# Attention stage of a fused three-layer kernel: g_norm multiplied on VectorE, a second set of q/k/v buffers, weight pieces summed after a batch's additions

## What is computed

```python
kv = np.einsum('bhsd,bhse->bhde', k, v)          # per head, 64 x 64
out = np.einsum('bhsd,bhde->bhse', q, kv)
rms = np.sqrt(np.mean(out * out, axis=-1, keepdims=True) + 1e-06)
x = out / rms * g_norm                            # heads side by side: x is (8, 576, 512)
mixed = np.real(fft(fft(x, axis=1), axis=2))
u = x + mixed
# layer 1: u + relu(layernorm(u) @ w_ch1) @ w_ch2; layer 2: a mix over the sequence by U, V, then the same without the norm
```

## Time and profile before

| | |
|---|---|
| median of 3 runs | 1843.4 us (1842.77 to 1852.18) |
| profiled execution | 1847.24 us, span 1844.9 us |
| PE busy | 1744.3 us (95%), mean granted clock 0.983 |
| DVE busy | 1376.6 us (75%) |
| POOL busy | 612.4 us (33%) |
| ACT busy | 784.6 us (43%) |

### The profile page before, as it was taken

How to read it: one execution, slowest core, us unless ns; L and a number is a source line. 1 busy time by engine, 2 the same in 40 slices (tenths; PEclk the granted TensorE clock), 3 DMA queues, 4 the chain that set the end, 5 groups by cost and what they waited for, 6 DMA issues and landing times.

```text
span 1844.9 us, 25843 instructions
## 1 busy us (share of the span) xinstructions
PE 1744.3 (95%) x9908; PEld 1677.4 (91%) x9908; DVE 1376.6 (75%) x1559; ACT 784.6 (43%) x1126; POOL 612.4 (33%) x428
## 2 busy tenths in 40 slices
PE   6889879989999999999999999799999999999998
PEld 5667768979999999999999999699999999999998
DVE  4779987997777877867966868956956857758667
ACT  2333343544544544445444436334334334443442
POOL 2888973351231330330410313620400402303203
PEclk9889989999999999999999999899999999999999
DMA  7487557988787787887876779776766766767663
GB/s 254 157 277 247 203 206 272 336 326 279 261 300 270 276 290 258 293 283 254 289 250 239 259 235 344 287 262 237 242 240 232 251 227 238 249 224 247 230 244 120
DMA packets 123819, 470.04 MB, mean 255 GB/s; under 512 B 12273, under 2 KB 49649, under 8 KB 84018
## 3 DMA queue, kind: packets, MB, share of 16 engines
q1 hardware_dynamic: 122482, 467.21, 71.9%
q10 hardware_dynamic: 1216, 1.18, 0.2%
HBM read 389.70 MB, written 78.64 MB: 254 GB/s over the span
## 4 chain that ended last, share of the span: by engine, by line
PE 75%; DVE 12%; issue 4%; POOL 4%; DMA 3%; ACT 1%; SPq 1%; DVEq 0%; POOLq 0%; ACTq 0%
PE pair L841 11%; PE pair L843 11%; PE pair L842 11%; PE pair L858 11%; PE pair L860 11%; PE pair L859 11%; DVE t_raw L1370 2%; DVE t_lo L1351 2%; PE tr_ps L725 2%; PE pair L632 2%; DMA in_sb<-x_dram 1%; PE pair L653 1%; DVE w_sb L1283 1%; POOL t_raw L1576 1%; DVE eo_sb L1241 1%
## 5 line engine op out<-in xcount | busy, mean ns | idle before, releaser
L858 PE MATMUL pair<-t_hi,w_sb 128*128 128x384 f32 x1344 | 462.1, 344 | 34.2 <-DVE t_lo L1351 34.2
L841 PE MATMUL pair<-t_hi,w_sb 128*128 128x384 f32 x1344 | 460.5, 343 | 7.9 <-DVE h_sb L1388 7.1
L859 PE MATMUL pair<-t_lo,w_sb 128*128 128x384 f32 x1344 | 457.4, 340 | 0.0
L860 PE MATMUL pair<-t_hi,w_sb 128*128 128x384 f32 x1344 | 457.2, 340 | 0.0
L843 PE MATMUL pair<-t_hi,w_sb 128*128 128x384 f32 x1344 | 455.6, 339 | 0.0
L842 PE MATMUL pair<-t_lo,w_sb 128*128 128x384 f32 x1344 | 455.5, 339 | 0.0
L1351 DVE TENSOR_TENSOR t_lo<-t_raw,t_hi 128x768 fp32r<-128x768 f32 x300 | 345.4, 1158 | 13.5 <-ACT t_hi L1070 10.0
L1576 POOL TENSOR_TENSOR t_raw<-h_sb 128x768 f32<-128x768 f32 x60 | 152.0, 2534 | 575.5 <-PE pair L860 575.5
L1085 ACT ACTIVATE t_hi<-t_raw 128x768 fp32r<-128x768 f32 x240 | 202.2, 846 | 318.9 <-DVE t_raw L1370 239.4
L858 PEld LDWEIGHTS pair<-t_hi,w_sb 128*128 128x128 f32 x1344 | 254.3, 189 | 42.6 <-DVE t_lo L1351 42.3
L841 PEld LDWEIGHTS pair<-t_hi,w_sb 128*128 128x128 f32 x1344 | 252.6, 188 | 15.6 <-issue 10.2
(11 more groups left out here) (149 smaller groups left out, 2104.9 us busy)
## 6 DMA issues: line engine op xcount, KB each, us to landing
w_sb<-wc SPq DMA_DIRECT2D x260, 1024.0 KB, 4.9
wc<-w_sb SPq DMA_DIRECT2D x28, 1024.0 KB, 5.8
w_raw<-wr1a SPq DMA_DIRECT2D x24, 512.0 KB, 4.6
w_raw<-wr1b SPq DMA_DIRECT2D x24, 512.0 KB, 4.2
wc<-pb SPq DMA_DIRECT2D x16, 640.0 KB, 4.9
w_raw<-wr2a SPq DMA_DIRECT2D x10, 1024.0 KB, 7.0
wc<-pb_v SPq DMA_DIRECT2D x16, 640.0 KB, 5.2
w_raw<-wr2b SPq DMA_DIRECT2D x10, 1024.0 KB, 6.8
```

What stands on the lines that cost most here:

```text
L841: nc.tensor.matmul(ps, w_hi, hi[:, x, :], start=(fresh and x == 0), stop=False, skip_group_check=True)
L858: nc.tensor.matmul(ps, w_hi, hi[:, f, :], start=(fresh and k == 0 and f == 0), stop=False, skip_group_check=True)
L859: nc.tensor.matmul(ps, w_hi, lo[:, f, :], start=False, stop=False, skip_group_check=True)
L860: last = nc.tensor.matmul(ps, w_lo, hi[:, f, :], start=False, stop=(k == 3 and f == 1), skip_group_check=True)
```

## The change

It does three things. DVE does the multiplication by g_norm itself, directly behind each group's `normalise`, as two instructions of 96x512 in place on x_sb; POOL's `weigh` is gone. k, v and q have two sets of buffers, used by turns, and the loads wait for the last reader of two batches ago instead of the last batch; the place of the loads in SP's list changes with it: in the loop of batch b now k, v and q of b come first, then the weight pieces, then `store_u(b-2)`. Weight pieces are summed on POOL behind the batch's additions, two each for b = 1, 2, 3 and one each for b = 4, 5; ACT rounds them in the next step behind `copy_g`, DVE makes the remainder at the end of that step, and SP stores them in the loop after (`MOVED`).

```diff
+    sets = (base + 31744, base)
+    k_sb = [at(f"k_sb{r}", sets[r], [128, 5, D]) for r in range(2)]      # v_sb, q_sb alike
-        SUM_MIDDLE, SUM_END = {1: 0, 2: 2, 3: 4, 4: 5, 5: 6, 6: 7}, {1: 1, 2: 3}
-        SPLIT_EARLY, SPLIT_END = {2: 1, 3: 3}, {1: 0, 2: 2, 3: 4, 4: 5, 5: 6, 6: 7}
-        MOVED = {2: (0, 1), 3: (2, 3), 4: (4,), 5: (5,), 6: (6,), 7: (7,)}
+        SUMMED = {1: (0, 1), 2: (2, 3), 3: (4, 5), 4: (6,), 5: (7,)}
+        MOVED = {b + 2: units for b, units in SUMMED.items()}
 SP
             def load_kv(b):
+                r = b % 2
+                if b >= 2:
+                    sp.wait_ge(kv_summed, b - 1)
...
             def load_q(b):
+                if b >= 2:
+                    sp.wait_ge(att_done, 2 * NT * (b - 1))
...
-            next_kv(2)
-            load_unit(UNITS[1])
             for b in range(2, B):
-                next_q(b)
-                if b < B - 1:
-                    next_kv(b + 1)
-                for n in MOVED[b]:
+                load_kv(b)
+                load_q(b)
+                for n in MOVED.get(b, ()):
                     store_unit(UNITS[n])
                     if n + 2 < 8:
                         load_unit(UNITS[n + 2])
                 if b == 6:
-                    for q in range(NCH):
+                    for q in range(4):
                         load_in(q)
                 store_u(b - 2)
+            sp.wait_ge(att_done, 2 * NT * (B - 1))
+            for q in (4, 5):
+                load_in(q)
             store_u(B - 2)
 ACT, phase1_step(b)
-                if b in SPLIT_EARLY:
-                    split_unit_hi(UNITS[SPLIT_EARLY[b]])
                 copy_seq(b - 1, (0, 1))
                 root(b, 1)
                 copy_seq(b - 1, (2, 3))
                 copy_g(b - 1)
+                for n in SUMMED.get(b - 1, ()):
+                    split_unit_hi(UNITS[n])
                 square(b, 2, False)
...
-                if b in SPLIT_END:
-                    split_unit_hi(UNITS[SPLIT_END[b]])
 DVE, normalise(b, g)
+                for m in range(2):
+                    dve.wait_ge(scaled, 2 * (NT * b + g) + m + 1)
+                    x = x_sb[b % 3][:, 2 * g + m, :].rearrange("p (h e) -> p h e", h=H)
+                    nc.vector.tensor_tensor(x, x, gn_sb[:, :].unsqueeze(1).to_broadcast([PT, H, HD]), ALU.mult).then_inc(x_ready, 1)
 DVE, end of phase1_step(b)
-                if b in SPLIT_END:
-                    split_unit_lo(UNITS[SPLIT_END[b]])
+                for n in SUMMED.get(b - 1, ()):
+                    split_unit_lo(UNITS[n])
 POOL
-            def weigh(b, g):
...
             for b in range(1, B):
-                weigh(b, 0)
-                weigh(b, 1)
-                if b in SUM_MIDDLE:
-                    sum_unit(UNITS[SUM_MIDDLE[b]])
-                weigh(b, 2)
                 for t in range(NT):
                     add_transform(b - 1, t)
-                if b in SUM_END:
-                    sum_unit(UNITS[SUM_END[b]])
+                for n in SUMMED.get(b, ()):
+                    sum_unit(UNITS[n])
```

More of the change, by code:

```diff
@@ L183, in build_program @@
     o = base
-    k_sb = at("k_sb", o, [128, 5, D])
-    v_sb = at("v_sb", o + 10240, [128, 5, D])
-    q_sb = at("q_sb", o + 20480, [128, NP, 2 * NT * PT])
     kv_sb = at("kv_sb", o + 29696, [128, NP, 128])
[L188 to L191, removed]
+    sets = (base + 31744, base)
+    k_sb = [at(f"k_sb{r}", sets[r], [128, 5, D]) for r in range(2)]
+    v_sb = [at(f"v_sb{r}", sets[r] + 10240, [128, 5, D]) for r in range(2)]
+    q_sb = [at(f"q_sb{r}", sets[r] + 20480, [128, NP, 2 * NT * PT]) for r in range(2)]
     w_sb = [at(f"w_sb{r}", base + 8192 * r, [128, 2, 4, 2, 128], F32R) for r in range(RING)]
@@ L302, in build_program @@
         kv0_loaded, q0_loaded = [sem(f"kv0_loaded{n}") for n in range(2)], sem("q0_loaded")
-        kv_loaded, q_loaded = sem("kv_loaded"), sem("q_loaded")
+        kv_loaded, q_loaded = [[sem(f"{what}_loaded_{r}") for r in range(2)] for what in ("kv", "q")]
         kv_zeroed, warm_zeroed = sem("kv_zeroed"), sem("warm_zeroed")
@@ L404, in load_kv @@
             def load_kv(b):
[L405 to L408, removed]
+                r = b % 2
+                if b >= 2:
+                    sp.wait_ge(kv_summed, b - 1)
+                sp.dma_start(k_sb[r][:, 0:4, :], k_main[b]).then_inc(kv_loaded[r], 16)
+                sp.dma_start(k_sb[r][0:64, 4, :], k_rest[b]).then_inc(kv_loaded[r], 16)
+                sp.dma_start(v_sb[r][:, 0:4, :], v_main[b]).then_inc(kv_loaded[r], 16)
+                sp.dma_start(v_sb[r][0:64, 4, :], v_rest[b]).then_inc(kv_loaded[r], 16)
             def load_q(b):
-                sp.dma_start(q_sb[:, :, :], q_t[b]).then_inc(q_loaded, 16)
+                if b >= 2:
+                    sp.wait_ge(att_done, 2 * NT * (b - 1))
+                sp.dma_start(q_sb[b % 2][:, :, :], q_t[b]).then_inc(q_loaded[b % 2], 16)
             def load_unit(unit):
@@ L428, in _ @@
                 cols = slice(256 * n, 256 * (n + 1))
-                sp.dma_start(k0_sb[:, 0:4, cols], k_main[0][:, :, cols]).then_inc(kv0_loaded[n], 16)
-                sp.dma_start(k0_sb[0:64, 4, cols], k_rest[0][:, cols]).then_inc(kv0_loaded[n], 16)
-            sp.dma_start(q0_sb[:, :, :], q_t[0]).then_inc(q0_loaded, 16)
+                sp.dma_start(k_sb[0][:, 0:4, cols], k_main[0][:, :, cols]).then_inc(kv0_loaded[n], 16)
+                sp.dma_start(k_sb[0][0:64, 4, cols], k_rest[0][:, cols]).then_inc(kv0_loaded[n], 16)
+            sp.dma_start(q_sb[0][:, :, :], q_t[0]).then_inc(q0_loaded, 16)
             sp.dma_start(gn_sb[:, :], g_norm.partition_broadcast(PT)).then_inc(gn_loaded, 16)
@@ L440, in _ @@
             load_unit(UNITS[0])
[L442 to L448, removed]
+            load_unit(UNITS[1])
             def store_u(b):
@@ L621, in _, with kv_products @@
         def _(pe):
-            def kv_products(b, k_sb=k_sb, v_sb=v_sb, very_first=False):
-                if not very_first:
-                    pe.wait_ge(kv_loaded, 64 * b)
+            def kv_products(b):
+                r = b % 2
+                if b:
+                    pe.wait_ge(kv_loaded[r], 64 * ((b + 1) // 2))
                     pe.wait_ge(kv_copied, 2 * b)
                 for h in range(NP):
-                    if very_first and h % 2 == 0:
+                    if b == 0 and h % 2 == 0:
                         pe.wait_ge(kv0_loaded[h // 2], 64)
@@ L631, in kv_products, with attention @@
                         rows = 128 if t < 4 else 64
-                        last = nc.tensor.matmul(kv_ps[:, cols], k_sb[0:rows, t, cols], v_sb[0:rows, t, cols],
+                        last = nc.tensor.matmul(kv_ps[:, cols], k_sb[r][0:rows, t, cols], v_sb[r][0:rows, t, cols],
                                                 start=(t == 0), stop=(t == 4))
                 last.then_inc(kv_summed, 1)
-            def attention(b, groups, first, late=False, q_sb=q_sb):
+            def attention(b, groups, first, late=False):
                 if 0 in groups:
@@ L640, in attention @@
                     else:
-                        pe.wait_ge(q_loaded, 16 * b)
+                        pe.wait_ge(q_loaded[b % 2], 16 * ((b + 1) // 2))
                     pe.wait_ge(kv_copied, 2 * (b + 1))
@@ L653, in attention @@
                             last = nc.tensor.matmul(ps[0:PT, 128 * h:128 * (h + 1)],
-                                                    q_sb[:, h, PT * (2 * g + m):PT * (2 * g + m + 1)],
+                                                    q_sb[b % 2][:, h, PT * (2 * g + m):PT * (2 * g + m + 1)],
                                                     kv_sb[:, h, :], start=True, stop=True)
@@ L714, in phase1_step @@
                 feature_transform(b - 1, first)
-            kv_products(0, k0_sb, v0_sb, very_first=True)
-            attention(0, (0, 1), True, q_sb=q0_sb)
+            kv_products(0)
+            attention(0, (0, 1), True)
             kv_products(1)
-            attention(0, (2,), True, q_sb=q0_sb)
+            attention(0, (2,), True)
             for b in range(1, B):
@@ L1012, in phase1_step @@
                 copy_cos(b - 1, 2, first)
-                if b in SPLIT_END:
-                    split_unit_hi(UNITS[SPLIT_END[b]])
             for n in range(2):
                 cols = slice(256 * n, 256 * (n + 1))
-                act.dma_start(v0_sb[:, 0:4, cols], v_main[0][:, :, cols]).then_inc(kv0_loaded[n], 16)
-                act.dma_start(v0_sb[0:64, 4, cols], v_rest[0][:, cols]).then_inc(kv0_loaded[n], 16)
+                act.dma_start(v_sb[0][:, 0:4, cols], v_main[0][:, :, cols]).then_inc(kv0_loaded[n], 16)
+                act.dma_start(v_sb[0][0:64, 4, cols], v_rest[0][:, cols]).then_inc(kv0_loaded[n], 16)
             act.wait_ge(warm_zeroed, 1)
@@ L1229, in normalise @@
                         ALU.mult).then_inc(scaled, 1)
+                if b == 0 and g == 0:
+                    dve.wait_ge(gn_loaded, 16)
```

(8 more changed lines are left out.)

2 lines of the change are left out of this document (removed).

## The result

The changed kernel takes 1930.6 us (median of 4 runs, 1925.3 to 1932.0) against 1847.8 us for the kernel before (median of 4 runs): a ratio of 1.044 (95% interval 1.041 to 1.047), 83 us slower. Each kernel has one profile, so a difference of a few us between single steps rests on one execution. The direction and the mechanism were forecast; the size was not: 1900 us, range 1868 to 1925.

The account below looks back on a forecast made before the run. DVE was taken to pace the steady step. Terms of -0.7, -1.6, +11.6, +18.5, +18.5, +12.2 and -1.9 summed to +56.6 us on 1847.2, giving 1903.8, then 1900 for the median; range 1868 to 1925.

Parts of the forecast that it names:

- part 2: Place of the loads in SP's list: k and v come late, changing steps 2 to 6 by -1.6, +11.6, +18.5, +18.5, +12.2 us.
- rival B: First stage: k and v in time, ACT's wait for the weight pieces decides; 1843 us, as before; 5%.
- step 7: Stretch between marks without kv products, where only the multiplication's gain counts: -1.9 us.
- T: Time from the kv products' start to the step's mark: 15.5 us plus 2.2 for PE's slower clock, 17.7.
- K: Offset in a step at which k and v have landed: 16.5, 28.5 (three times) and 22.5 us in steps 2 to 6.
- landing: Time from the issue of k_main to v_rest, with u in front and q behind: 12 us, bounds 9.8 and 15.2.
- I add 2.2: Allowance in T for PE's lower clock after waiting for k and v: 2.2 us, bounds 0 and 3.3.
- The offset of k_main: When SP issues the first k load within a step: 4.8, 16.5 (three times) and 8.4 us in steps 2 to 6.
- the tail: Last stretch of the first stage, ahead of the channel layers: 15.5 us, forecast unchanged.
- The high case of the sum: Upper bound for the kernel: landing 15.2 us and the clock's cost at 3.3 us, +20, 1920 us.
- Rival D: q, issued right behind, shares DMA engines with v_rest: K of 33 in steps 3 to 5, 1915 to 1930 us; 12%.
- part 1: Multiplication on DVE: in a steady step 5.9 us back for 3.6 paid, about 25.5 us where DVE bounds it.

Follow-up runs that it names:

- e1: Changed kernel with k, v and q of the next batch issued ahead of the weight pieces and u stores; 1854.0 us.
- e3: Changed kernel with PE doing 46 to 88 filler matmuls while it waits for k and v; 1932.3 us.
- e4: Changed kernel with the next batch's k, v and q issued behind the weight pieces but ahead of the u stores; 1893.4 us.
- e5: Changed kernel with q issued only once k and v of its batch have landed, from batch 3 on; 1922.6 us.
- e6: Kernel before with only the multiplication moved from POOL to DVE; 1846.4 us, ratio 0.997.
- e8: As e2, but where two pieces come in one step, DVE makes the second remainder behind the next step's normalise; 1836.9 us.
- e2: As e1, with ACT rounding the weight pieces at the end of its step instead of behind copy_g; 1840.7 us.
- e9: As e3 with fewer filler matmuls (29, 56, 66, 61 and 54); 1920.7 us.

## Why the prediction was off

Right by the runs: that SP passes the pieces and the u stores before k and v (part 2), in all five steps; that the waits on the two sets themselves hold nothing; that ACT's wait for the pieces hides under the late k and v and comes out when they are in time (rival B: e1 lies at 1854, no different from before, with steps of 37.8 and 37.5, where the prediction had 37); step 7 (26.9 for 26.2); T of 15.5 us where the clock is up (e3).

Wrong was the size of the terms of K + T. Issue, landing, K and T of the changed kernel, with what the prediction had in brackets:

| step | k_main issued at | landing | K | T | length |
|---|---|---|---|---|---|
| 2 | 3.9 (4.8) | 13.4 (11.7) | 17.3 (16.5) | 20.9 (17.7) | 38.2 (34.0) |
| 3 | 18.2 (16.5) | 14.5 (12) | 32.7 (28.5) | 19.8 (17.7) | 52.5 (46.2) |
| 4 | 18.2 (16.5) | 15.4 (12) | 33.6 (28.5) | 17.3 (17.7) | 50.9 (46.2) |
| 5 | 18.1 (16.5) | 14.1 (12) | 32.2 (28.5) | 21.2 (17.7) | 53.3 (46.2) |
| 6 | 8.5 (8.4) | 15.6 (14.1) | 24.1 (22.5) | 17.7 (17.7) | 41.8 (40.2) |

- Landing, +11.3 us over the five steps, the largest. The step "here u is in front and q behind: 12" took a value between the two rows. The row behind u and q, 15.2 us, was the nearer one: u stands in front in both, and e4 shows that it counts (10.8 to 11.7 without u in front), e5 that q behind adds 1.0.
- T, +8.4 us. "I add 2.2 (bounds 0 and 3.3)": the clock cost 5.4, 4.3, 1.8, 5.7 and 2.2 us. The bound was read from groups of six matmuls; here all 40 records of the kv products (6 us of work at full speed) lay behind a wait of up to 17 us, and in steps 2 and 5 all ran at the lower level, 11.0 us. Two rows that the prediction had gave the higher bound: 6.0 us for the 40 records, doubled as the six of the earlier trace rows are (3.26 for 1.62), is up to 6 us more.
- The offset of k_main, +4.1 us (5.0 in steps 3 to 6, -0.9 in step 2). In passing the pieces the second store, with a load in front, took 7.1 us to land (112.72 to 119.83), not 5.8, and the u stores 2.8 us of SP's time, not 2.3.

With the tail (16.8 for 15.5) and the channel layers (1576.3 us for 1579.4) these terms make up the 78.5 us between the two spans: 56.6 forecast, +23.8 from the table, +0.2 rounding in step 2, +0.7 in step 7, -0.7 ahead of step 2, +1.2 in the tail, -3.1 in the layers, 78.7 in all.

The last step of the sum failed as well: "the median of the runs is 3.8 lower" than the profiled execution, which turned 1903.8 into 1900. The 3.8 came from three runs; the median of the changed kernel lies 5.3 us above its profiled execution (1930.6 and 1925.3), and that of before, with a fourth run, 0.6 above. Of the 30.6 us between 1900 and 1930.6 this is 9, the terms of the stage and the layers are the rest.

The range failed by 6 us at its upper end. The high case of the sum, 1920, did take landing at 15.2 and the clock at 3.3 together. Landing stayed within that (+11.3 of some +14), so what carried the time past it were the bound of the clock, 3.3 where up to 5.7 were lost, the passing of the pieces, which had no bound, and the step from profile to median. Rival D (K of 33, 1915 to 1930) lies nearest to the measured case, K of 32.2 to 33.6, but by luck: it was named for q, which e5 shows to be the smallest part of the landing.

In part 1 the steady step was forecast at 25.5 us; e1, e6 and e8 have 26.4. Half of the 0.9 us is the price of the multiplication, six times 0.68 (its median) or 4.1 us for the 3.6 taken; the other half was not followed. The gain from moving 84 us of work off POOL is 1.3 us a step where nothing else waits, and 0 to 0.5% of the kernel (e6).

## What to carry to other kernels

A second set of buffers gives nothing by itself: when a load is issued is decided by the queue's program order, so ask of each load what the issuing engine must pass first, and at what offset its reader is due. Put loads ahead of stores and of anything that waits for this step's results. A wait for a late source inside one engine's list (a rounding, a sum, a store that must land) delays everything behind it, and it shows only once the longer wait that covers it has gone.

## What the runs showed of the hardware

- A wait of PE is often paid twice. In e2 a gap of 2.7 us was followed by four groups at the lower level, 12.4 us from the first start to the last end where e8 takes 6.5; there the gap at the same place is 1.3 us and the clock stays up. The filled waits of e3 show the same products at 6.0 us that took 7.8 to 11.0 behind a gap.
- The length of the gap alone does not tell the price. In e9 a gap of 2.7 us before the same group (155.02 us) left it at full speed, 1.73 us for six records; in the changed kernel the products took 11.0 us behind the shortest wait (7.3 us) and 7.8 us behind the longest (17.1 us).
- The 1 MB and 128 KB transfers of k and v take 9.8 us with little in flight, 10.8 to 11.7 behind weight pieces (e4, steps 3 to 5), 14.1 to 15.4 with 1.2 MB of u stores in front as well; the last two have 1.2 MB of q behind them, which adds 1.0.
- The start of a run varies: the kv products of batch 0 took 9.0 us in one piece in the changed kernel, and in e3 were held 4.5 us in the middle by v_rest, with the first mark 9 us later. So the time of e3's profile holds 9 us that are not its edit's; how much of the spread of the other times this makes was not followed.
